# Attention step of a fused kernel: slots of two pairs of heads placed between the two turns of x, and loops of two rounds written out

## The reference

```python
B, H, S, Ns, D = (8, 8, 512, 32, 64)
def _attn_ref(x, state):                       # x [B,H,S,D], state [B,H,Ns,D]
    scores = scale * np.matmul(x, state.transpose(0, 1, 3, 2))
    a = softmax(scores)                        # over the 32 states
    xread = np.matmul(a, state)
    scores2 = scale * np.matmul(state, x.transpose(0, 1, 3, 2))
    a2 = softmax(scores2)                      # over the 512 rows of x
    sread = np.matmul(a2, x)
    return np.concatenate([xread, sread], axis=2)
```

## Time and profile before

| | |
|---|---|
| median of 3 runs | 1315.77 us (1315.48 to 1319.13) |
| time of the profiled execution | 1321.82 us |
| its span on the core | 1320.1 us |
| granted TensorE clock | 1.00 of full speed, all through |
| PE busy | 1304.0 us (99%), 6381 matmuls |
| DVE, ACT, POOL busy | 953.5, 410.2, 384.4 us |
| DMA | 113.44 MB, 86 GB/s in the mean |

### The profile page before, as it was taken

One profiled execution on the slowest core, in us unless ns is written; L12 is line 12 of the kernel. 1 busy time (PEld: TensorE's weight loads), 2 busy tenths in 40 slices (PEclk: granted clock), 3 DMA queues, 4 the chain that ended last, 5 costly groups with the idle time before them and its releaser, 6 DMA issues.

```text
span 1320.1 us, 20465 instructions
## 1 busy us (share of the span) xinstructions
PE 1304.0 (99%) x6381; PEld 1087.7 (82%) x6382; DVE 953.5 (72%) x2036; ACT 410.2 (31%) x641; POOL 384.4 (29%) x212
## 2 busy tenths in 40 slices
PE   8999999999999999999999999999999999999998
PEld 7888888888788888888888888888888888888887
DVE  4666889898889898957767577675775766757344
ACT  3455322222222222332222222222222222222232
POOL 2377462966690939370010100100101001001010
PEclk9999999999999999999999999999999999999999
DMA  7856545665964546730010100000101001000000
GB/s 169 249 153 183 163 139 135 157 174 142 195 146 125 151 112 239 191 115 17 16 40 16 40 17 17 34 18 12 40 16 40 16 16 40 16 8 33 0 33 17
DMA packets 104575, 113.44 MB, mean 86 GB/s; under 512 B 49232, under 2 KB 68688, under 8 KB 104016
## 3 DMA queue, kind: packets, MB, share of 16 engines
q1 hardware_dynamic: 62928, 64.57, 18.0%
q10 hardware_dynamic: 35136, 30.42, 8.9%
q0 software_dynamic: 6464, 17.86, 3.6%
HBM read 69.80 MB, written 43.02 MB: 85 GB/s over the span
## 4 chain that ended last, share of the span: by engine, by line
PE 95%; DMA 1%; DVE 1%; issue 1%; ACT 1%; another core or an unknown queue 0%; ACTq 0%; SPq 0%; DVEq 0%
PE area L1852 28%; PE area L1866 28%; PE area L1801 16%; PE area L1756 16%; PE area L1570 2%; PE area L1540 2%; PE area L1560 1%; PE area L1527 1%; DMA xin<-in_x 1%; PE area L1594 1%; PE area L1587 1%; DMA st_diag<-in_state 0%; ACT W L687 0%; SPq L383 0%
## 5 line engine op out<-in xcount | busy, mean ns | idle before, releaser
L1852 PE MATMUL area<-ys,W 128*128 128x512 f32 (+1 forms) x1728 | 394.1, 377 | 0.0
L1866 PE MATMUL area<-W,gs 128*128 128x512 f32 x1632 | 393.5, 389 | 0.0
L1852 PEld LDWEIGHTS area<-ys,W 128*128 128x128 f32 x1728 | 313.3, 188 | 61.1
L1866 PEld LDWEIGHTS area<-W,gs 128*128 128x128 f32 x1632 | 305.3, 188 | 62.9 <-DVE gs L1422 0.2
L1323 DVE STREAM_TRANSPOSE area<-hrow 32x256 f32<-32x256 f32 x576 | 262.6, 456 | 38.1 <-ACT hrow L785 29.5
L860 ACT ACTIVATE gate<-gate,half_col 128x512 f32<-128x512 f32 (+1 forms) x144 | 100.7, 700 | 376.5 <-DVE gate L1412 374.8
L1801 PE MATMUL area<-W,hs 128*128 x888 | 209.7, 392 | 1.1 <-issue 1.1
L1412 DVE TENSOR_SCALAR gate<-area 128x512 f32<-128x512 f32 (+1 forms) x144 | 95.3, 662 | 159.3 <-PE area L1852 159.1
L662 POOL DMA_INDIRECT out<-orow,out_row x32 | 30.8, 963 | 592.5 <-ACT orow L876 504.2
L1756 PE MATMUL area<-W,xs 128*128 x864 | 201.9, 389 | 0.0
L1801 PEld LDWEIGHTS area<-W,hs 128*128 128x128 f32 x888 | 165.2, 188 | 41.4 <-issue 8.1
(11 more groups left out here) (218 smaller groups left out, 802.8 us busy)
## 6 DMA issues: line engine op xcount, KB each, us to landing
stage<-in_moe_w SPq DMA_DIRECT2D x64, 256.0 KB
stage<-in_moe_w SPq DMA_DIRECT2D x16, 1024.0 KB
sorted_y<-ytile ACTq DMA_DIRECT2D x38, 256.0 KB
tile_y<-ytile ACTq DMA_DIRECT2D x38, 256.0 KB
xtile<-slot_x ACTq DMA_DIRECT2D x144, 64.0 KB
yrow<-sorted_y SPq DMA_DIRECT2D x32, 256.0 KB, 2.7
xin<-in_x SPq DMA_DIRECT2D x60, 128.0 KB, 3.0
stage<-in_moe_w_in SPq DMA_DIRECT2D x4, 1024.0 KB
```

Source lines behind the costliest of these rows:

```text
L1852: last = nc.tensor.matmul(HIDDEN[n % 2][:, 0:width], wq[:, wp, :], ys[par][:, yp, k, 0:width], start=(k == 0 and wp == HI and yp == HI), s ...
L1866: last = nc.tensor.matmul(SUMS[a], gs[n % 2][:, gp, a * P:(a + 1) * P], W[:, q // 2 + 2, wp, at:at + DM], start=(n == 0 and gp == HI and w ...
```

## The change

On PE the turns of p2 come directly behind the turns of x's first half, read 3 behind them, and the slots of pairs 0 and 1 behind read 3, ahead of the turns of x's second half, with their wait for ACT's copy of p2. On ACT the copy of p2 goes ahead of the weight copy. The loops of the attention stage on PE (three rounds) and on ACT, DVE and POOL (two rounds each) become Python loops, so that their bodies are emitted once per round and step numbers are constants. No operation is added or taken away.

```diff
@@ POOL
-            with pool.Fori(1, B // 2 - 1) as m:
+            for m in range(1, B // 2 - 1):
@@ ACT
             def step(s, par, reuse=None, unit=None):
 
                 copy_x(0, PAIRS * s + 1)
+                copy_p2(s - 1)
                 if unit:
                     split_first(*unit)
-                copy_p2(s - 1)
                 copy_x(2, PAIRS * s + 3)
                 softmax(s, par, reuse)
...
-            with act.Fori(1, B // 2 - 1) as m:
+            for m in range(1, B // 2 - 1):
@@ DVE
-            with dve.Fori(1, B // 2 - 1) as m:
+            for m in range(1, B // 2 - 1):
@@ PE
                 for j in range(2):
                     transpose_x(j, par)
-                pe.wait_ge(xread_copied[1], 2 * r + 1)
-                read_rows(r, 3)
                 pe.wait_ge(prob2_done, b + 1)
                 pe.wait_ge(xread_copied[0], 2 * r + 2)
                 turn_p2(other)
+                pe.wait_ge(xread_copied[1], 2 * r + 1)
+                read_rows(r, 3)
+                pe.wait_ge(p2_copied, b + 1)
+                slots_rows(other, 0).then_inc(x_half_used, 1)
                 pe.wait_ge(xin_loaded[par][1], 16 * HALF * in_turn)
                 pe.wait_ge(xread_copied[0], 2 * r + 1)
                 for j in range(2, PAIRS):
...
                 pe.wait_ge(prob_done, b + 1)
                 pe.wait_ge(xread_copied[1], 2 * r + 2)
                 turn_p(other)
-                pe.wait_ge(p2_copied, b + 1)
-                slots_rows(other, 0).then_inc(x_half_used, 1)
                 pe.wait_ge(onehot_done, r + 1)
                 pe.wait_ge(tally_done, r + 1)
                 rank_rows(ranks(CH), par, CH, par)
...
-            with pe.Fori(1, B // 2) as m:
+            for m in range(1, B // 2):
```

## The result

The changed kernel takes 1319.24 us (median of 20 runs, 1318.61 to 1322.14), the kernel before on the same chip 1316.13 (20 runs, 1315.24 to 1319.13): ratio 1.0021, interval 1.0015 to 1.0028. That is 3.1 us slower, inside the 0.3% that I had set as the bound of "no change", but on the other side of 1.000 than the forecast of 1312.8 us, and 0.24 us above the top of the range, 1319.0.

The account below looks back on a forecast made before the run. PE was taken to bound the kernel; steps of 15.36 us work plus 0.52, 0.36 and 0.07 of new waits make steps 3 to 7 81.6 against 84.6 us, gaining 3.0: 1312.8 us, range 1309.5 to 1319.0.

Parts of the forecast that it names:

- part 1: PE, between turns of x's second half and scores: waits for x and xT copies vanish, 7.8 us over steps 3 to 7.
- No change: Rival, 20%: late signals may belong to the profiled execution only; steps of 15.8 to 16 us against 16.3; 1315 to 1316.
- Parts 2 and 3: New PE waits each step: turns of p2 for DVE's scaling of prob2T, 0.52 us; slots for ACT's copy of p2, 0.36.
- part 4: PE's turns of scores lose cover for ACT's copy of the scores: wait 0.07 us a step, bounds 0 and 0.2.
- More: Rival, 15%: new waits mostly smaller, by half in each of six steps, because straight code issues sooner; 1309.8 us.
- Part 5: DVE's choice of experts, read 3 and POOL's division are moved but still covered; counted as nothing.
- Part 6: Attention loops written out: costed at nothing, bounded by a gain or loss of at most 0.1 us a step.
- slower rival: Rival, 15% for three or more steps: the turned p2 is signalled late, delaying the slots 3.25 us a step; up to 1329.
- two late signals: Two steps in which the signal of turned p2 comes late, 3.25 us each; gain gone, 1316.3; counted under no change.
- S + 7.9: Sign: ACT's copy of p2 comes about 6.9 + 1.0 us behind the start of the turns of scores.
- S to S: Sign: an attention step, from one start of the turns of scores to the next, takes 16.3 us.

Follow-up runs that it names:

- e1: The kernel before, unchanged, measured and profiled again: 1315.64 us, ratio 1.0004 to before.
- e5: The changed kernel with DVE scaling prob2T before it copies read 1: 1317.33 us, ratio 1.0012 to before.
- e6: The changed kernel with the slots of pair 1 moved back behind the turns of p: 1317.07 us, ratio 1.0014 to before.
- e7: The changed kernel with both prob2T scaled before read 1 is copied and the slots of pair 1 moved back: 1315.67 us, ratio 1.0000 to before.
- e3: The kernel before with only the new order on PE and ACT, loops kept: 1319.35 us, ratio 1.0030 to before.
- e2: The kernel before with only the four loops written out, old order: 1315.84 us, ratio 1.0007 to before.
- e12: The kernel before, unchanged, profiled again on a chip where it is slower: 1320.02 us, ratio 0.9998 to before.

## Why the prediction was wrong

**The step that failed is in part 1: "I take all 7.8 us as gone".** Of these 7.8 us of waiting in steps 3 to 7, about half are not in an ordinary run (e1, on a chip where before takes 1315.19 us against 1316.13 here). With 15.36 us of work a step, the 80.45 us of e1 hold 3.7 us of waiting in those five steps, and the new order puts 6.0 us of its own in place (82.76 less 76.8). That is 2.3 us lost in five steps, against 3.1 measured in the whole kernel. On chips C and D, where before takes 1320 to 1321.5 us (on D with 83.05 us in the steps), the same change is even. The prediction carried the profile's saving over to the median with "the same difference gives 1312.8 us"; this sentence was the error. The evidence against it stood beside it: the profiled time lay 2.7 us above the slowest of the runs shown.

**The rival "No change" had it right and was priced wrong.** It said that the late signals may belong to the profiled execution and put an ordinary step at 15.8 to 16 us against 16.3. Measured: 16.09 (e1's mean) against 16.53. A difference of 0.3 to 0.5 us a step over the six steps of the new order is 2 to 3 us *slower*, 1318 or 1319; I wrote 1315 to 1316, as if the waits for x came on top, although the 16 us of such a step hold them (2.5 us in e1). Worked out properly it would have been the rival on the slower side, and deserved more than 20%.

**Parts 2 and 3 held.** Turns of p2: forecast 0.52, measured 0.44. Slots: forecast 0.36, measured 0.40, and 0.11 more because the 16 slots take 1.89 us behind a wait and 1.78 without; that term I did not have. e5 took out the wait of part 2, e6 that of part 4 and e7 both: the step fell by 0.39, 0.29 and 0.67 us. With the loops kept the wait of part 2 is 0.56 us (e3), so the rival "More" had a grain of truth, 0.12 us of its 0.44 a step.

**Part 4 was mis-sized**: 0.07 forecast (bounds 0 and 0.2), 0.26 measured. It took the end of the scores from the chain of the earlier trace rows, where ends of matmuls are modelled, and the cover from differences of starts in the timeline. Both from starts: ACT's copy begins 0.20 us behind the start of the turns of p (110.27 and 110.47), takes 1.01, and the turns of scores start 1.27 behind (111.54), against 1.01 of cover. Step 2 of the first profile had the 0.20 already: turns of p at 41.93, and in the timeline of ACT:

```profile
42.13 1.01 ACT L699 COPY prob<-area 128x1024 f32<-128x1024 f32 x1 [3.37 <-PE area L1540]
```

**Part 5 held**: no wait of PE is put down to the choice of experts or to POOL's division, and the six steps take 16.42 to 16.65 us. **Part 6 held** in the medians (e2, ratio 1.0007); in e2's trace it is 0.2 us a step, above the bound of 0.1. **The slower rival did not occur**: the turned p2 is signalled in time on every chip, C and D too; ACT's copy stands 1.08 to 1.20 us behind its turns in all four traces of the changed kernel. Its sum was wrong as well: two late signals of 3.25 us on top of 1312.8 give 1319.3 and not 1316.3, so the range up to 1319.0 did not take them in as it said. Of the signs listed, the pieces' order, the unbroken 4.4 us of turns and scores, the missing waits for x and the copy at S + 7.9 came true; S to S was 16.53 and not 16.3. One of the signs of being wrong came too: a difference behind the attention stage, 1.8 us between the two traces.

**Even against its own trace the sum was off**: forecast 84.6 to 81.6, measured 84.56 to 82.76, so 1.8 us of the 3.0, or 0.2 us a step short, nearly all of it part 4 and the slow start of the slots. The span agreed (3.0 us) by chance: 1.8 us of it lie in the steps, 1.8 behind the attention stage, where the change does nothing and the chips differ (below), and 0.6 were lost ahead of step 3.

Put in one sentence: slots 0 and 1 had been the cover of ACT's copy of the scores, read 3 that of DVE's scaling of prob2T, and the turns of x's second half, the scores and the turns of p that of ACT's copy of p2; the change spent all three to cover the loads of x and the copies of xT, and where these are not late it buys 0.7 us a step for 1.2.

**What stays open**: why DVE and ACT see PE's signals late on chips C and D and not on A, B and E; what besides the place of POOL's indirect DMAs it takes (the loads of x and of weights that run at the same time were not varied); and where on C and D the 0.3 to 3 us more behind the attention stage go. The medians differ by chip, but single runs of the kernel before on the first chip (1319.13) and on A (1319.66) are as long as those on C and D, so that the chip may not be all that decides. Whether the lateness differs between the cores of one chip was not tried.

## What to carry to other kernels

Before a change is built on the waits of one profile, hold the profiled execution's own time against the spread of the runs: where it lies outside, as 1321.82 did over 1315.48 to 1319.13, its largest irregular waits (these came in some steps and not in others, with a releaser that the trace could not name) may not be in the runs at all, and the sum has to be made without them too. For every piece that is moved, ask first which wait it was covering at its old place; in a stretch in which PE is busy for 94 to 97% each of them may cover something, and the price of baring a copy is the whole copy plus its signals (here 1.27 us from start to start for 128x1024 f32) less what still stands between. Where a piece waits for several transfers at once, waiting by parts costs one semaphore and no cover: with both halves by pairs and the loops written out it gained 0.23% on two chips and was not slower on the third.

## What was not expected of the hardware

The kernel before, at a granted clock of 0.998 to 1.000 everywhere, took 1315.2 to 1316.1 us on some chips and 1320.2 and 1321.5 on two others. Two things make up most of it. Behind the attention stage, where all kernels here are alike, it takes 1188.8 to 1189.4 us on A, B and E and 1189.7 to 1191.8 on C and D. And in the attention stage DVE and ACT start later behind a PE group on C and D: DVE's copy of xT up to 2.8 us behind the start of the eight turns in e12, 2.0 in its rows above, against 1.1 to 1.7 on A; such a late copy begins 0.8 to 1.2 us after POOL's fourth indirect DMA has ended (e12 and the first trace). The changed kernel has no such late copy on any chip, so its 1.1 to 2.4 us more on C and D (1321.31 and 1320.33 against 1319.24 and 1318.90) go with the first part: 1191.2 and 1191.1 us from S of step 7 to the end, against 1189.0 and 1189.2.
